# Reordering one group's triangular inversion in a delta-rule attention and mixture-of-experts kernel

## The reference

```python
# q, k, v: (2, 8, 768, 48); beta: (2, 8, 768)
k_n = k / (norm(k) + 1e-6)
for t in range(S):                       # delta rule: one step per token
    y[t] = q[t] @ state
    v_old = state.T @ k_n[t]
    state = state + beta[t] * outer(k_n[t], v[t] - v_old)
# layer 2, 1536 tokens x 384:
h = x @ w_in                             # 384 -> 1024
solu = h * softmax(h)
x = layer_norm(solu, g_ln) @ w_out       # 1024 -> 384
# layer 3: top-1 of 8 experts, relu(x @ w1[e]) @ w2[e], scaled by the gate's probability
```

## Time and profile before

| | |
|---|---|
| median of 3 runs | 432.77 us |
| profiled execution, its own time | 432.51 us |
| its span | 430.8 us |
| TensorE (PE) busy | 392.6 us, 91% |
| VectorE (DVE) busy | 303.5 us, 70% |
| ScalarE (ACT) busy | 228.1 us, 53% |
| GpSimd (POOL) busy | 66.1 us, 15% |
| mean granted TensorE clock | 0.969 of full |

### The profile page before, as it was taken

The page is one execution under the profiler, slowest core; times in us unless marked ns, Lnnn a source line. Parts: engine busy times, 40 slices in busy tenths (PEclk is TensorE's granted clock), DMA queues, the critical chain, the costliest instruction groups (busy, mean ns, idle before and its releaser), DMA issues.

```text
span 430.8 us, 13183 instructions
## 1 busy us (share of the span) xinstructions
PE 392.6 (91%) x5507; PEld 373.5 (87%) x5508; DVE 303.5 (70%) x601; ACT 228.1 (53%) x410; POOL 66.1 (15%) x80
## 2 busy tenths in 40 slices
PE   3878897998779999999999998999999999999992
PEld 3878896797769888999887998999999999999991
DVE  5899576799957687993416987796596685647650
ACT  2556443778141137653125972577586594638550
POOL 3101100000020000001020000625134243210211
PEclk9999999999967999999999997999999999999997
DMA  6998003950100148001028801245827739180000
GB/s 154 309 211 216 5 3 81 219 219 20 38 2 22 22 99 179 19 22 40 5 59 275 329 37 39 59 169 201 310 80 289 259 111 317 26 310 22 27 3 26
DMA packets 25574, 52.00 MB, mean 121 GB/s; under 512 B 4468, under 2 KB 19120, under 8 KB 25040
## 3 DMA queue, kind: packets, MB, share of 16 engines
q1 hardware_dynamic: 21216, 44.95, 33.6%
q0 software_dynamic: 3136, 4.73, 3.6%
q10 hardware_dynamic: 1168, 1.52, 1.7%
HBM read 44.30 MB, written 9.44 MB: 125 GB/s over the span
## 4 chain that ended last, share of the span: by engine, by line
PE 72%; DVE 17%; issue 4%; ACT 3%; POOL 0%; ACTq 0%; POOLq 0%; DVEq 0%
PE PS L571 10%; PE PS L573 10%; PE PS L572 10%; PE PS L1675 8%; PE PS L1529 4%; PE PS L1581 3%; PE PS L1594 3%; DVE Tm L1088 3%; PE PS L1722 2%; PE PS L1541 2%; PE PS L1732 2%; PE PS L1555 2%; PE PS L1723 2%; PE PS L1448 2%; DVE Tw L1091 2%
## 5 line engine op out<-in xcount | busy, mean ns | idle before, releaser
L571 PE MATMUL PS<-xTh,w1h 128*128 128x224 f32 (+3 forms) x198 | 55.7, 282 | 0.6 <-DVE hTl L480 0.6
L573 PE MATMUL PS<-xTh,w1l 128*128 128x224 f32 (+3 forms) x198 | 55.5, 280 | 0.0
L572 PE MATMUL PS<-xTl,w1h 128*128 128x224 f32 (+3 forms) x198 | 55.5, 280 | 0.0
L1675 PE MATMUL PS<-w_in_h,mlpT 128*128 128x512 f32 x144 | 46.5, 395 | 2.5 <-ACT mlpT L872 1.5
L571 PE MATMUL PS<-w2h,hTh 128*128 128x384 f32 x136 | 46.1, 339 | 0.0
L573 PE MATMUL PS<-w2h,hTl 128*128 128x384 f32 x136 | 45.5, 335 | 0.0
L572 PE MATMUL PS<-w2l,hTh 128*128 128x384 f32 x136 | 45.5, 334 | 0.0
L571 PEld LDWEIGHTS PS<-xTh,w1h 128*128 128x128 f32 x198 | 37.9, 191 | 1.0 <-DVE hTl L480 1.0
L480 DVE SCALAR_TENSOR_TENSOR hTl<-PS,hTh 128x384 fp32r<-128x384 f32 x64 | 35.4, 553 | 4.7 <-ACT hTh L378 4.7
L506 POOL DMA_INDIRECT out<-yo,oiu x24 | 24.0, 1000 | 92.6 <-ACT yo L389 84.6
L573 PEld LDWEIGHTS PS<-xTh,w1l 128*128 128x128 f32 x198 | 37.9, 192 | 0.0
(11 more groups left out here) (194 smaller groups left out, 914.6 us busy)
## 6 DMA issues: line engine op xcount, KB each, us to landing
w1r<-w SPq DMA_DIRECT2D x8, 1536.0 KB, 6.5
w2r<-w SPq DMA_DIRECT2D x8, 1536.0 KB
KP<-kv SPq DMA_DIRECT2D x3, 1536.0 KB, 12.0
out<-zero SPq DMA_DIRECT2D x12, 192.0 KB, 3.7
x<-rowst SPq DMA_DIRECT2D x12, 192.0 KB, 1.9
QT<-qt SPq DMA_DIRECT2D x5, 384.0 KB, 6.4
yx<-yx SPq DMA_DIRECT2D x12, 144.0 KB, 2.5
XE<-w_out_t SPq DMA_DIRECT2D x1, 1536.0 KB, 6.5
```

The costliest lines, as they stand in the source:

```text
L571: pe.matmul(out_ap, lhs[0], rhs[0], start=first, stop=False)
L572: pe.matmul(out_ap, lhs[0], rhs[1], start=False, stop=False)
L573: return pe.matmul(out_ap, lhs[1], rhs[0], start=False, stop=final)
L1675: last = pe.matmul(PS[:, h_bank(g, n) + s, :], mlpT[:, n, x, c, :], w[:, c, o], start=(c == 0 and j == 0), stop=(c == KD - 1 and j == 2))
```

## The change

- VectorE, attention of group 0: `scales(1)` and `lower(1)` stand directly behind `mask_first`; the three fold steps stand two places to six places earlier; `rows_of_t(1)`, `(2)`, `(3)` follow them within the attention, where before only `(1)` did, at its end.
- VectorE, MLP of group 0: `rows_of_t` is split into `row_products` and `row_sums`; step 4 stands ahead of and behind the first maximum, step 5 around a `mlp_lo`; `place_factors(1)` stands ahead of `mlp_lo` of the last tile, `place_rows(1)` between its two halves.
- `lower_rows` of group 1: ScalarE copies one block, VectorE the other (as in group 0 before), with the semaphore `d_tb` for GpSimd and TensorE.
- ScalarE, group 0: `x_high` of tiles 0 and 1 ahead of the last `take_y` and its DMAs; `x_high` of tiles 2 and 3 ahead of the first `mlp_exp`.
- TensorE, group 0: `between(1)` ahead of the high half of the last `mlp_down`, `lower_block(1)` ahead of its low half.
- TensorE, prologue: 3 warm products in place of the last 6.

```diff
@@ GpSimd, clear_t; the same condition in TensorE's lower_block
-                    if g == 0:
-                        pool.wait_ge(d_tb, 1)
+                    if g < 2:
+                        pool.wait_ge(d_tb, g + 1)
@@ ScalarE, lower_rows
-                    for c in range(1 if g == 0 else 2):
+                    for c in range(1 if g < 2 else 2):
@@ ScalarE, first_attention
                     state(0, 3)
+                    x_high(0, 0)
+                    x_high(0, 1)
                     take_y(0, 3)
                     move_x(0, 1, row_pieces()[PIECES - 2:PIECES])
-                    x_high(0, 0)
-                    x_high(0, 1)
                     odd_blocks(2)
                     cross_blocks(2)
@@ ScalarE, mlp
-                    mlp_exp(g, 0)
+                    if g:
+                        mlp_exp(g, 0)
                     x_high(g, 2)
                     x_high(g, 3)
+                    if g == 0:
+                        mlp_exp(g, 0)
                     mlp_center(g, 0)
@@ VectorE: rows_of_t(b) = row_products(b) + row_sums(b), and
+                def lower_rows(g):
+                    dve.wait_ge(td_ready, g + 1)
+                    dve.tensor_copy(TT64[block(3), :, 1], TT64[block(3), :, 0]).then_inc(d_tb, 1)
@@ VectorE, first_attention
                     mask_first()
+                    scales(1)
                     solution(0, 1)
+                    lower(1)
+                    fold_steps(3)
                     query(0, 0, 1)
                     step_matrix(0, 0, 1)
-                    scales(1)
+                    fold_steps(2)
                     state(0, 0)
-                    lower(1)
+                    fold_steps(1)
                     query(0, 1, 0)
...
                     state(0, 2)
-                    fold_steps(3)
+                    rows_of_t(1)
                     state(0, 3)
-                    fold_steps(2)
+                    rows_of_t(2)
                     x_low(0, 0)
                     x_low(0, 1)
-                    fold_steps(1)
+                    rows_of_t(3)
                     systems(2)
-                    rows_of_t(1)
@@ VectorE, first_mlp
+                    row_products(4)
                     mlp_max(0, 0)
                     x_low(0, 2)
+                    row_sums(4)
                     mlp_mul(0, 0)
...
                     mlp_lo(0, 0, 0)
+                    mlp_lo(0, 0, 1)
                     mlp_mul(0, 2)
-                    mlp_lo(0, 0, 1)
                     mlp_max(0, 3)
-                    rows_of_t(2)
                     mlp_lo(0, 1, 0)
-                    rows_of_t(3)
+                    row_products(5)
                     mlp_lo(0, 1, 1)
+                    row_sums(5)
                     mlp_mul(0, 3)
-                    rows_of_t(4)
+                    rows_of_t(6)
                     mlp_lo(0, 2, 0)
-                    rows_of_t(5)
                     mlp_lo(0, 2, 1)
                     mask_scores(1, 0)
-                    rows_of_t(6)
+                    rows_of_t(7)
+                    place_factors(1)
                     mlp_lo(0, 3, 0)
-                    rows_of_t(7)
+                    place_rows(1)
+                    lower_rows(1)
                     mlp_lo(0, 3, 1)
-                    place_factors(1)
-                    place_rows(1)
                     scale_v(1)
@@ TensorE, mlp
                     mlp_down(g, 3, 0)
-                    if ahead and g:
+                    if g == 0:
+                        between(g + 1)
+                    elif ahead:
                         lower_block(g + 1)
                     mlp_down_high(g, 3, 1)
                     if not ahead:
                         more_counts()
                     if g == 0:
-                        between(g + 1)
+                        lower_block(g + 1)
                     mlp_down_low(g, 3, 1)
-                    if g == 0:
-                        lower_block(g + 1)
@@ TensorE, prologue
                 lower_block(0)
-                warm_products(6)
+                warm_products(3)
```

More of the change, by code:

```diff
@@ L1081, in rows_of_t, with row_products @@
                 def rows_of_t(b):
+                    row_products(b)
+                    row_sums(b)
+                def row_products(b):
                     j = ST * b
@@ L1089, in rows_of_t, with row_sums @@
                     link(dve.tensor_tensor(t[:, :, 0:2], t[:, :, 0:2], t[:, :, 2:4], ALU.add))
+                def row_sums(b):
+                    j = ST * b
+                    n = BL - 1 - j
+                    r = slice(j + 1, BL)
+                    t = Tm[:, 0:n * ST * j].rearrange("p (i l k) -> p i l k", l=ST, k=j)
                     for l in range(2):
@@ L1305, in _ @@
                 place_rows(0)
-                dve.wait_ge(td_ready, 1)
-                dve.tensor_copy(TT64[block(3), :, 1], TT64[block(3), :, 0]).then_inc(d_tb, 1)
+                lower_rows(0)
                 scale_v(0)
@@ L1507, in lower_block @@
                     pe.wait_ge(e_tb, g + 1)
-                    if g == 0:
-                        pe.wait_ge(d_tb, 1)
+                    if g < 2:
+                        pe.wait_ge(d_tb, g + 1)
                     pe.wait_ge(e_m1, g + 1)
```

## The result

The changed kernel took 421.09 us (median of 4; 419.82 to 423.88) against 435.34 us before on the same chip (median of 4; 432.31 to 439.6): ratio 0.9732, 95% interval 0.9692 to 0.9772. The ratios and their intervals leave out executions in a slower state, here the one of 439.6 us; the two raw medians stand 3.3% apart. Two later comparisons of the same two kernels gave 0.9625 (0.9580 to 0.9671) and 0.9695 (0.9674 to 0.9715). The forecast was 418.5 / 432.5 = 0.968. So the change is worth 2.7 to 3.75%, by the comparison taken; the profiled executions, 432.51 and 419.91 us, differ by 12.6 us.

What follows compares the result with a forecast made beforehand. VectorE was taken to bound the second half of group 0's MLP, with a low clock behind it. Sum: -0.9 - 1.3 - 9.1 - 2.7 = -14.0; 432.5 - 14.0 = 418.5 us, 8-in-10 range 416 to 423.2.

Steps and rivals of the forecast that it cites:

- point 6: Group 0's MLP: row steps gone, VectorE in time for `between`; 45.6 us in place of 54.7, -9.1 us.
- 1 and 4: Prologue: three fewer warm products, -0.9 us; first up product: `x_high` of tiles 0 and 1 before last `take_y`, -1.3 us.
- 2 and 3: Attention of group 0: VectorE's `scales`, `lower`, fold steps and row steps 1 to 3 fit around its idle gaps.
- rival B: Steps moved into the attention do not fit and push queries, states, first maximum; +6, 424.5 us; chance 0.08.
- 5: `x_high` of tiles 2 and 3 before the first exponential: first `mlp_mul` at 81.0 for 82.8, VectorE 1.8 us earlier.
- the yardstick from group 1: Group 1's MLP, same tasks with VectorE not late: 44.67 us from first up product to next solve, against 54.67 in group 0.
- 7: Clock stays at its upper level with TensorE's idle stretches gone; the solve of group 1 saves 2.7 us.
- rival A: The clock still falls between 110 and 125 us; about 422 us; chance 0.12.
- Rival C: Clock falls in the first attention for want of three warm products; 422.7 us; chance 0.07.

Runs made afterwards that it cites:

- warm6: The changed kernel with six warm products again in place of three; ratio 0.9693 to the kernel before, beside 0.9625 for the changed kernel.
- table_early: The changed kernel with a small exponential on ScalarE ahead of `odd_blocks(2)`, so the activation table loads there; ratio 0.9687 to the kernel before.
- x_high_back: The changed kernel with ScalarE's `x_high` of tiles 0 to 3 back in their old places; ratio 0.9786 to the kernel before.
- dve_alone: The kernel before with VectorE's new lists alone, without `lower_rows(1)`, all other engines as before; ratio 0.9853 to the kernel before.
- pe_order_back: The changed kernel with TensorE's old order at the end of group 0's MLP (`between`, `lower_block` later); ratio 0.9804 to the kernel before.
- before_kept_clock: The kernel before with products of zeros in TensorE's waits at the end of group 0's MLP; ratio 0.9923 to the kernel before.

## Why the prediction came out as it did

The mechanism was right in the main and the time lies in the stated range; the saving was put too high, 14.0 us (3.2%) against 12.6 between the profiled executions and 2.7% (0.9692 to 0.9772 as a ratio) in the timed runs. The two later comparisons lie on the forecast's either side. By the marks 0.1 us of the miss is at the first up product, 0.6 in the stage, 0.3 in the attention and MLP of group 1, and 0.3 in the tail.

The step that failed is point 6, the stage: it was put at -9.1 and measured -8.5. It held VectorE's end against `between` alone and took every other hand-over from group 1, where VectorE is not late. Point by point:

1 and 4. First solve: -1.4 measured, -0.9 forecast. First up product: -2.06 measured, -2.2 forecast. The wait for x is gone, but the gap without a releaser just ahead of it is 1.31 us in place of 0.79. I had taken the gaps of the trace as fixed; the list fixes where they stand, but their lengths at this one run from 0.79 to 1.34 us. That point 1 is worth something is shown by warm6.

2 and 3. The steps in the attention fit: TensorE has no new wait on VectorE there, and rival B did not come.

5. The first `mlp_mul` is at 81.5 (forecast 81.0), the exponential at 80.21 (79.9). The exponential again follows the table load at once (78.92 + 1.28 = 80.20), so the drain of the Trainium skill's page ("ScalarE: Activation LUTs", section "What ACT_TABLE_LOAD costs") shows neither here nor in table_early, where the next instruction also comes 0.01 us behind the load; the measurement decides.

6. Stage -8.5, forecast -9.1: the mis-sized term, 46.14 us for 45.6. Two waits of 0.53 and 0.24 us at `mlp_down`, which the yardstick from group 1 doesn't have, were left out: I checked VectorE only at `between` and not at each hand-over on the way. The wait for the copy out of `lower_block` is 0.6 beyond what the low products cover, where 0.9 was expected. The 2 us of slack that the step gave VectorE at `between` are no slack of the stage, since `mlp_lo` behind `place_factors` holds TensorE up just before: x_high_back passes on all of 2.1 us and table_early all of 0.8. That VectorE alone would bring nearly all of it, as dve_alone's expectation had it, fell: its list brings 6.0 us of the stage and 6.1 at the solve of group 2. Read at that last mark in the same way, ScalarE's two moves are worth 2.4 us on the kernel before and 2.4 to 3.0 in the changed one, TensorE's order 2.1 to 2.7, the warm products 0.2 to 0.8, the shared rows nothing that shows. With VectorE's 6.1 this makes 10.8 to 12.6 of the 13.0 us; each is read from one profile, and profiles of one kernel differ by 0.6 there.

7. The clock: inflow follows the solve by 7.27 in place of 9.80, -2.5 (forecast -2.7). The step's reason was too simple. It said that with VectorE in time the clock stays up; pe_order_back has VectorE in time for `between` and loses the clock, with 0.9 us more waiting before the solve and 0.3 more before `lower_block`. So I now hold rival A to have been nearer than its chance of 0.12 says, and that the clock held was in part luck. Rival C did not come in any profile of the changed kernel. The rule of "TensorE: Matmul & The Clock Gate" (Trainium skill, section "What's actually happening"), that activity lifts the throttle, fits before_kept_clock and the two kernels with an order put back; that fewer dummy products could only hurt did not hold here, since they stood in the way of work: from 44 to 50 us the granted clock is 1.00 with three and with six, and with six (warm6) the solve of group 2 is 0.2 to 0.8 us later.

The last sentence of the working was also too strong: "Nothing later in the program is changed, and what follows is TensorE's own work." In the two first profiles the tails are alike (230.6 and 230.9 us), but in three profiles of the changed kernel they are 230.9, 236.9 and 233.3 us, and some of that is waiting. A gain of 13 us at the solve of group 2 is therefore seen as 12.8 to 14.5 us between the medians of the three comparisons and as 2.7 to 3.75% in their ratios. What makes the tail differ is shown in part (the gather's wait on one chip, a gap without a releaser with low clock behind it in group 2); what sets off the one or the other in an execution stays open.

## What to carry to other kernels

Take a neighbouring repetition of the same stage in which the suspected engine is not late as the yardstick: it gave the stage to 0.6 us in 55. Then hold the suspected engine against every hand-over on the way, not only against the last: here two small waits in between were missed. A wait of TensorE of a microsecond can have a second price, the clock behind it; when the parts of a change are sized singly, look at the clock in each. When an engine comes earlier, subtract what was already there at the start of the stage: table_early's 1.4 us were 0.8. Compare stages between marks in the profile before believing a total: here the stage repeated to 0.02 us while the profiled span moved by 5.

## What the runs showed of the hardware

Gaps without a releaser on TensorE stand at fixed places of its instruction list (six passes taken out moved one by six passes), and last 0.79 to 1.34 us at about the same place in different kernels, 1.04 to 1.31 in three profiles of one. What causes them is not shown. The granted clock fell in x_high_back after two stretches in which TensorE worked 0.96 of 2 us each, at a place where it held in the first profile of the kernel before, which idled 0.79 and 1.26 us there: about as much in all (2.05 us for 2.08). The activation table load took 1.28 us each time, and the next activation could start 0.01 to 0.02 us behind it. From the issue of the first gather to the first use of its rows by ScalarE it was 4.9 us on one chip and 7.1 on another.
